# The first tile of each expert stage is started before its routing tables exist

## The chip, the cores and the metric

The kernel runs on 1 core of one Trainium2 chip. The metric is the device time of one execution in microseconds (us), as the median of several runs. Engines: PE is TensorE, DVE is VectorE, ACT is ScalarE, POOL is GpSimd, SP is the sync engine, which here only issues DMAs.

## The reference, cut to what matters

Three stages follow one another: a linear attention over 4 x 768 tokens, then a mixture of 8 experts, then a second mixture of 8 experts that takes the first one's output.

```python
x = attention(r, k, v, w, u)                   # 3072 tokens x 384
# first mixture: cosine logits; second mixture: plain logits, and a sigmoid gate besides
expert_idx = np.argmax(logits, axis=1)
for e in range(E):                             # E = 8
    mask = expert_idx == e
    h = np.maximum(x[mask] @ w1[e], 0.0)       # 384 -> 1024
    out[mask] = gate_w[mask, None] * (h @ w2[e])   # 1024 -> 384
```

A token goes to one expert. So each mixture needs the tokens sorted by expert, and the second one can't know the places of its tokens until the first has ended.

## The kernel before, in words

**Attention.** 24 units (6 chunks of 128 positions x 4 batch rows). After each chunk, DVE works out for its 512 tokens the expert (`norms1`, `choose1`, L815 to L837) and the place of each in a DRAM table `sorted1` (`place1`, L839 to L861). POOL then scatters the rows there with four indirect DMAs (`tokens`, `scatter`, L403 to L415). The last chunk's turn comes after the last unit.

**Tables.** From the totals per expert DVE builds a table of tiles (`tables`, L873 to L901): for each tile of 128 rows its expert, its offset in `sorted1`, and where the next expert's weights go. SP writes 128 padding rows behind the last row of each expert (`pads`, L308 to L313). ACT, DVE, PE and POOL wait on `tabs[m]` for the table of mixture m.

**Expert stage.** One tile is one round of a hardware loop. For tile g: ACT loads the 128 rows into `xin` (`load_rows`, L643), PE transposes them (`transpose_x`, L1291), ACT and DVE split the result in a high and a low part (`copy_xt` L650, `rest_xt` L1027), PE multiplies with the first weights (`first_product`, L1302 and L1307), ACT applies the relu (L654), PE transposes (`transpose_h`, L1317), ACT and DVE split again (`copy_ht` L659, `rest_ht` L1032), PE multiplies with the second weights (`second_product_hi` L1328, `second_product_lo` L1336), and DVE scales by the gate (`gated`, L1043). In round p, PE does `transpose_h(p)`, `first_product(p+1)`, the second product of p and `transpose_x(p+2)`. There are 27 tiles in either mixture. In mixture 1 (m = 0) each output tile is also routed for mixture 2: `transpose_y`, `logits_y`, `ranks_y` on PE, `choose` and `place_row` on DVE (L980 to L1013), and an indirect DMA into `sorted2` on POOL.

**Weights.** An expert's weights come in six pieces of 512 KB (`load_raw`, SP, L303), each into a buffer of its own. ACT writes the high part (`split_hi`, L554, about 1 us a piece) and DVE the low part (`split_lo`, L863, 1.2 us a piece); then SP may load the next expert's piece into that buffer. The first three pieces (`SOON`) hold the first weights, the last three (`LATE`) the second ones. `with_next_expert` splits `SOON` in the round of an expert's first tile and `LATE` one round later.

**The fallback.** If a test on `w` fails, all engines take a long branch (`If(bad > 0)`) that recomputes the attention in another way. The test's flag is ready at `fl_ready`. On these inputs the branch is not taken. On DVE it stands behind `tables(0)`.

The order on an engine is that of the program text, and the start of a stage reads, on ACT:

```python
act.dma_start(xin[:, :], (sorted1, sorted2)[m][0:P, :])   # after all rows have landed and the first pads
act.sem_inc(mo["ext"], 1)
act.wait_ge(tabs[m], 1)
act.wait_ge(pads_done[m], 16 * E - 16)
copy_xt(0)
load_rows(1)
```

Of the kernel before, what the change touches and what calls it, by code (L numbers as in the profile page):

```python
# [15 lines left out]
P = 128  # L16
# [53 lines left out]
def build(nc, rk_in, w_in, v_src, seq_in, uflat_in, upair_in, emb_in, epair_in, vT_in, tau_in, wall1_in, wg2_in, wall2_in, out):  # L70
# [4 lines left out]
    with ExitStack() as ctx:  # L75
# [54 lines left out]
        slot2 = sb("slot2", [P, 1], I32)  # L130

# [65 lines left out]
        pad0_done = [sem(f"pad0_done{m}") for m in range(2)]  # L197
# [7 lines left out]
        gp_chain, dve_chain, redo_chain = sem("gp_chain"), sem("dve_chain"), sem("redo_chain")  # L205
        fl_sum, fl_ps, fl_ready = sem("fl_sum"), sem("fl_ps"), sem("fl_ready")
# [59 lines left out]
        def _(sp):  # L266
# [35 lines left out]
            sp.wait_ge(gp_const, 1)  # L302
            def load_raw(k):  # L303
# [4 lines left out]
            def pads(m):  # L308

                sp.wait_ge(padaddr[m], 1)  # L310
                for e in range(E):
                    row = sp.value_load(padi[0:1, m, e:e + 1], min_val=e * CAP, max_val=e * CAP + N)
                    sp.dma_start((sorted1, sorted2)[m][bass.ds(row, P), :], padrow[:, :]).then_inc(pads_done[m] if e else pad0_done[m], 16)  # L313
# [6 lines left out]

            sp.wait_ge(fl_ready, 1)
            bad = sp.value_load(flag[0:1, 0:1], min_val=0, max_val=1)
            with sp.If(bad > 0):
# [22 lines left out]
                sp.wait_ge(padaddr[0], 2)  # L346
            with sp.Else():
                sp.nop()
            sp.nop()


            pads(0)
            for k in range(RAWS, 2 * E * RAWS):
                if k == (E + 2) * RAWS:
                    pads(1)
# [5 lines left out]
        def _(gp):  # L361
# [41 lines left out]
            def tokens(n, c, q):  # L403
                gp.wait_ge(rts[0]["slots"], n + 1)
                gp.wait_ge(row_copied, min(B * n + B, UNITS))
                gp.iota(rows[:, q, :, TOK], [[S, B]], base=c * C, channel_multiplier=1, allow_small_or_imprecise_dtypes=True).then_inc(toks, 1)
                gp.wait_ge(toks, n + 1)

# [38 lines left out]
            with gp.If(bad > 0):  # L447
# [3 lines left out]
                gp.wait_ge(tabs[0], 2)  # L451
# [32 lines left out]
        def _(act):  # L484
# [75 lines left out]
            def step(c, u, b, nu, nb):  # L560
# [18 lines left out]
                if u >= UNITS - RAWS:  # L579
                    split_hi(0, 0, u - UNITS + RAWS)  # L580
# [14 lines left out]

            LC = NCHUNK - 1
            copy_row(UNITS - 1, LC, B - 1)
# [7 lines left out]
            with act.If(bad > 0):  # L605
# [11 lines left out]
                act.wait_ge(tabs[0], 2)  # L617
# [21 lines left out]

            for m in range(2):  # L640
                mo = moes[m]

                def load_rows(g):  # L643
                    off = act.value_load(tab[0:1, m, bass.ds(g + TAB_OFF, 1)], min_val=0, max_val=SLOTS - P)
                    act.wait_ge(mo["ext"], g + 1)
                    act.dma_start(xin[:, :], (sorted1, sorted2)[m][bass.ds(off, P), :]).then_inc(mo["x_in"], 16)
# [14 lines left out]

                if m == 0:
# [3 lines left out]
                else:  # L666
                    act.wait_ge(moes[0]["sc"], 16 * last + 32)
                act.wait_ge(pad0_done[m], 16)
                act.dma_start(xin[:, :], (sorted1, sorted2)[m][0:P, :]).then_inc(mo["x_in"], 16)
                act.sem_inc(mo["ext"], 1)  # L670
                act.wait_ge(tabs[m], 1)
                last = act.value_load(tab[0:1, m, TAB_LAST:TAB_LAST + 1], min_val=E - 1, max_val=TILES - 2)
                act.wait_ge(pads_done[m], 16 * E - 16)
                copy_xt(0)
                load_rows(1)
                for n in range(2):
                    relu(0, n)
                copy_xt(1)
                load_rows(2)
                with act.Fori(0, last) as p:  # L680
                    copy_ht(p)
# [10 lines left out]
                    load_rows(p + 3)  # L692

                copy_ht(last)
                with_next_expert(act, m, last - 1, split_hi, LATE)
                if m == 0:
# [3 lines left out]
                    exps(last + 1)  # L700
                    copy_yt(last + 2)
                    keep_row(last + 2)
                    exps(last + 2)
                    with_next_expert(act, m, last, split_hi, LATE)
# [6 lines left out]
        def _(v):  # L711
# [13 lines left out]
            link(v.memset(St[:, :, :, :], 0.0))  # L725

# [49 lines left out]
            def step(c, u, b, nu, nb):  # L776
                par = b % 2

                def route():
                    if c > 0 and b == 2:  # L780
                        norms1(c - 1, c - 1)
                        choose1(c - 1)
                    if c > 0 and b == 3:
# [55 lines left out]
            def place1(n, c, q):  # L839
# [9 lines left out]
                v.wait_ge(rt["cnt"], n + 1)  # L849
                if n % NCHUNK == NCHUNK - 1:  # L850
# [575 lines left out]
```

## Time and profile before

| what | us |
| --- | --- |
| median of 3 runs | 814.78 |
| lowest and highest run | 814.62 and 816.25 |
| the profiled execution's own time | 813.74 |
| its span | 812.0 |
| PE busy | 732.1 (90% of the span) |
| DVE busy | 502.8 |
| ACT busy | 390.9 |

Times of instructions are counted from the start of the span. "Idle before" is the time for which an engine had nothing running before the instruction, with what released it behind the arrow; "issue" stands for nothing that the profile shows. A matmul at the granted clock of 1.00 runs at 2.4 GHz, at 0.50 at 1.2 GHz.

### The profile page before, as it was taken

What the parts mean: (1) busy time and instruction counts of PE and PEld (TensorE: products, weight loads), DVE (VectorE), ACT (ScalarE), POOL (GpSimd) and SP (SyncE); (2) the same over time, 40 slices, a digit from 0 to 9 for tenths busy, and PEclk for the clock granted to TensorE, in tenths of its full rate; (3) what the DMA queues carried; (4) which work ended last, traced back from release to release, by engine and by line L of the source; (5) the groups of instructions that cost most, each with busy time, mean ns of one, the idle gap of its engine ahead of it and who ended that gap; (6) DMA issues with size and microseconds to landing.
All of it is one profiled execution on the core that took longest, in us unless ns stands there. A gap on an engine that the chain in (4) does not pass through costs nothing.

```text
span 812.0 us, 21320 instructions
## 1 busy us (share of the span) xinstructions
PE 732.1 (90%) x5494; PEld 645.0 (79%) x5495; DVE 502.8 (62%) x1363; ACT 390.9 (48%) x760; POOL 159.9 (20%) x202
## 2 busy tenths in 40 slices
PE   3999899970899999999999998499999999999994
PEld 2787777760788889898888987379999999999993
DVE  7999998967467584746675665544635444436621
ACT  3666776680446463635464463144534444425521
POOL 5445565552000000000000000001000000010000
PEclk9999999895899999999999999789999999999997
DMA  6665788616433350423352433324605152415110
GB/s 130 161 160 142 203 250 232 168 61 211 181 128 116 117 183 31 150 75 109 117 178 87 141 116 117 100 88 136 202 29 194 47 184 79 157 39 194 39 33 27
DMA packets 50268, 103.75 MB, mean 128 GB/s; under 512 B 7921, under 2 KB 29904, under 8 KB 50224
## 3 DMA queue, kind: packets, MB, share of 16 engines
q1 hardware_dynamic: 29536, 67.18, 26.7%
q10 hardware_dynamic: 15568, 21.76, 10.0%
q0 software_dynamic: 5120, 14.26, 4.7%
q8 instruction: 23, 0.38, 0.2%
q14 instruction: 21, 0.17, 0.1%
HBM read 85.73 MB, written 19.01 MB: 129 GB/s over the span
## 4 chain that ended last, share of the span: by engine, by line
PE 70%; DVE 9%; issue 6%; ACT 5%; DMA 3%; ACTq 3%; SPq 1%; POOL 1%; DVEq 0%; POOLq 0%
PE bank L1302 18%; PE bank L1328 17%; PE bank L1336 10%; PE bank L1307 9%; PE bank L1317 5%; PE bank L1269 2%; ACT wall L558 2%; PE bank L1291 2%; DVE Q L755 2%; DVE SF L764 2%; DMA rk<-rk_in 2%; PE bank L1123 1%; PE bank L1110 1%; ACTq L503 1%; ACTq L245 1%
## 5 line engine op out<-in xcount | busy, mean ns | idle before, releaser
L1302 PE MATMUL bank<-wall,xT_hi 128*128 (+1 forms) x660 | 180.4, 409 | 3.0 <-ACT xT_hi L650 3.0
L1328 PE MATMUL bank<-wall,hT_hi 128*128 x880 | 165.6, 339 | 0.8 <-ACT hT_hi L659 0.5
L1328 PEld LDWEIGHTS bank<-wall,hT_hi 128*128 128x128 f32 x880 | 153.1, 188 | 7.9 <-issue 5.8
L868 DVE TENSOR_TENSOR wall<-raw,wall 128x1024 f32 (+1 forms) x96 | 112.0, 1221 | 61.9 <-ACT wall L558 58.6
L1302 PEld LDWEIGHTS bank<-wall,xT_hi 128*128 128x128 f32 x660 | 119.9, 192 | 23.9 <-issue 3.8
L654 ACT ACTIVATE hs<-bank 128x512 f32<-128x512 f32 x110 | 65.0, 591 | 110.9 <-PE bank L1307 103.8
L558 ACT ACTIVATE wall<-raw 128x1024 f32 (+1 forms) x96 | 95.0, 1050 | 42.0 <-issue 42.0
L1307 PE MATMUL bank<-wall,xT_lo 128*128 (+1 forms) x330 | 94.7, 395 | 0.0
L659 ACT ACTIVATE hT_hi<-bank 128x512 fp32r<-128x512 f32 x110 | 59.7, 595 | 70.7 <-PE bank L1317 70.7
L1336 PE MATMUL bank<-wall,hT_lo 128*128 x440 | 90.9, 348 | 0.0
L461 POOL DMA_INDIRECT sorted<-yrow,slot x28 | 27.3, 976 | 299.8 <-DVE yrow L1013 299.8
L1029 DVE TENSOR_TENSOR xT_lo<-bank,xT_hi 128x384 fp32r<-128x384 f32 x57 | 31.8, 558 | 86.9 <-ACT xT_hi L650 86.9
L475 POOL DMA_INDIRECT out<-ybuf,toki x28 | 27.3, 976 | 255.1 <-DVE ybuf L1054 255.1
L1336 PEld LDWEIGHTS bank<-wall,hT_lo 128*128 128x128 f32 x440 | 74.8, 189 | 0.0
L1307 PEld LDWEIGHTS bank<-wall,xT_lo 128*128 128x128 f32 x330 | 62.8, 190 | 14.4
L1035 DVE TENSOR_TENSOR hT_lo<-bank,hT_hi 128x512 fp32r<-128x512 f32 x110 | 70.9, 686 | 3.1 <-ACT hT_hi L659 1.6
L1317 PE MATMUL bank<-ident,hs 128*128 128x128 f32 x440 | 57.1, 272 | 1.0 <-ACT hs L654 1.0
L1317 PEld LDWEIGHTS bank<-ident,hs 128*128 128x128 f32 x440 | 51.2, 140 | 3.3 <-ACT hs L654 1.4
L1291 PE MATMUL bank<-ident,xin 128*128 128x128 f32 x171 | 28.8, 278 | 24.4 <-DMA xin<-sorted 24.4
L1110 PE MATMUL bank<-Rq,Kb 64*128 64x128 f32 x384 | 30.6, 304 | 19.6 <-DVE Kb L769 19.6
L1291 PEld LDWEIGHTS bank<-ident,xin 128*128 128x128 f32 x171 | 22.4, 143 | 31.8 <-DMA xin<-sorted 24.6
L1110 PEld LDWEIGHTS bank<-Rq,Kb 64*128 64x128 f32 x384 | 25.8, 204 | 23.6 <-issue 15.5
(194 smaller groups left out, 968.4 us busy)
## 6 DMA issues: line engine op xcount, KB each, us to landing
raw<-wall_in SPq DMA_DIRECT2D x96, 512.0 KB, 3.8
xin<-sorted ACTq DMA_DIRECT2D x59, 194.0 KB
rk<-rk_in SPq DMA_DIRECT2D x46, 192.0 KB
v_in<-v_src ACTq DMA_DIRECT2D x24, 192.0 KB, 4.3
vT<-vT_in ACTq DMA_DIRECT2D x48, 96.0 KB, 4.6
wb<-w_in SPq DMA_DIRECT2D x46, 96.0 KB
sorted<-padrow SPq DMA_DIRECT2D x16, 194.0 KB, 2.3
sorted<-yrow,slot POOLq DMA_INDIRECT x28, 2.7
```

The source lines that it names most:

```text
L558: act.activation(w_hi[:, slot, q * RAWC:(q + 1) * RAWC], raw[:, q], ACT.Copy).then_inc(w_his, 1)
L654: act.activation(hs[:, n * 512:n * 512 + 512], bank[n][:, :], ACT.Relu).then_inc(mo["h_sb"], 1)
L659: act.activation(hT_hi[:, 4 * n:4 * n + 4], bank[4 + n][:, :].rearrange("p (k t) -> p k t", k=4), ACT.Copy)\
L868: v.tensor_tensor(w_lo[:, slot, cols], raw[:, q], w_hi[:, slot, cols].bitcast(F32), ALU.subtract).then_inc(w_split, 1)
L1035: v.tensor_tensor(hT_lo[:, 4 * n:4 * n + 4], bank[4 + n][:, :].rearrange("p (k t) -> p k t", k=4), hT_hi[:, 4 * n:4 * n + 4].bitcast(F32), ...
L1110: last = pe.matmul(bank[hf][:, a * C:(a + 1) * C], Kb[q, k, a, :], Rq[q, k, a, :], start=True, stop=True, skip_group_check=True)
L1291: last = pe.transpose(bank[6][:, k * P:(k + 1) * P], xin[:, k * P:(k + 1) * P], ident[:, :])
L1302: pe.matmul(bank[n][:, :], xT_hi[:, k, :], w[:, bass.ds(slot, 1), cols].rearrange("p o n -> p (o n)"), start=(k == 0 and w is w_hi), stop= ...
L1307: last = pe.matmul(bank[n][:, :], xT_lo[:, k, :], w_hi[:, bass.ds(slot, 1), k * F + c0:k * F + c0 + 512].rearrange("p o n -> p (o n)"), st ...
L1317: last = pe.transpose(bank[4 + hf][:, j * P:(j + 1) * P], hs[:, n0:n0 + P], ident[:, :])
L1328: pe.matmul(bank[2][:, 0:DM], hT_hi[:, j, :], w[:, bass.ds(slot, 1), W2 + j * DM:W2 + (j + 1) * DM].rearrange("p o n -> p (o n)"), start=( ...
L1336: last = pe.matmul(bank[2][:, 0:DM], hT_lo[:, j, :], w_hi[:, bass.ds(slot, 1), W2 + j * DM:W2 + (j + 1) * DM].rearrange("p o n -> p (o n)" ...
```

## The change

What it does, in its parts:

- **First pads early.** SP writes padding into the first 128 rows of `sorted1` and `sorted2` at the start of the kernel.
- **Count of what the first tile needs.** In `place1` of chunks 1 to 4, DVE adds an instruction that counts for how many chunks the first expert had fewer than 128 tokens (`need`); in `place_row` it does the same for the tiles of mixture 1 (a new step 5). SP reads the counts (`need_ready`).
- **First tile.** SP, not ACT, loads the rows of tile 0 once the needed chunks or tiles have landed, without waiting for the tables. PE, ACT and DVE run all of tile 0, second product included, ahead of the wait on `tabs[m]`; the low part of its rows and of the `LATE` pieces of the first expert are made inside `tables`, behind its fifth instruction (`between`).
- **First round peeled.** The loop now starts at p = 1. What is left of round 0 stands ahead of it: load tile 1, split the `SOON` pieces of expert 1, `first_product(1)`, and so on.
- **Pads and raw weights by need.** SP issues the pads of experts 0 and 1, then raw pieces 6 to 8, waits for tile 1's rows, issues the other six pads, then the rest of the pieces. ACT waits for two pads ahead of `load_rows(1)` and for the other six ahead of `load_rows(2)`. For mixture 2, SP issues tile 0's load, all eight pads, waits for tile 1's rows, and goes on with the pieces.
- **Order.** `split_hi(0)` runs in units 16 to 21 and not 18 to 23. On DVE `split_lo(0)` runs in unit 23 and right behind it, ahead of the flag; the flag comes ahead of `norms1(5)`; the branch comes ahead of `tables(0)`. An extra Sqrt on ACT stands ahead of the last `copy_row`. POOL's iota no longer waits for `slots`.

```diff
@@ SP
+            sp.wait_ge(first_pad, 32)
+            for q in range(2):
+                for b in range(B):
+                    sp.wait_ge(landed[q][b], chunks[q])
+            sp.dma_start(xin[:, :], sorted1[0:P, :]).then_inc(moes[0]["x_in"], 16)
+            pads(0, range(2))
+            for k in range(RAWS, RAWS + len(SOON)):
+                sp.wait_ge(w_split, k - RAWS + 1)
+                load_raw(k)
+            sp.wait_ge(moes[0]["x_in"], 32)
+            pads(0, range(2, E))
+            for k in range(RAWS + len(SOON), 2 * E * RAWS):
+                if k == (E + 1) * RAWS + len(SOON):
+                    sp.wait_ge(need_ready[1], 1)
...
+                    sp.wait_ge(moes[0]["sc"], tiles)
+                    sp.dma_start(xin[:, :], sorted2[0:P, :]).then_inc(moes[1]["x_in"], 16)
+                    pads(1, range(E))
+                    sp.wait_ge(moes[1]["x_in"], 32)
                 sp.wait_ge(w_split, k - RAWS + 1)
                 load_raw(k)
@@ ACT
+            act.activation(en[:, 1:2], en[:, 0:1], ACT.Sqrt).then_inc(e_root, 1)
             copy_row(UNITS - 1, LC, B - 1)
...
+                act.sem_inc(mo["ext"], 1)
+                copy_xt(0)
+                for n in range(2):
+                    relu(0, n)
+                copy_ht(0)
                 if m == 0:
                     for q in range(2):
                         for b in range(B):
                             act.wait_ge(landed[q][b], 16 * NCHUNK // 2)
...
                 act.wait_ge(tabs[m], 1)
+                act.wait_ge(pad01_done[m], 32)
+                load_rows(1, ends[0:m])
...
+                act.wait_ge(mo["mm2"], 2)
+                for q in SOON:
+                    split_hi(E * m + 1, 1, q)
                 copy_xt(1)
+                act.wait_ge(pads_done[m], 16 * E - 32)
                 load_rows(2)
...
+                copy_xt(2)
+                load_rows(3)
+                copy_ht(1)
+                with act.Fori(1, last) as p:
@@ DVE, place1
+                if 0 < n < NCHUNK - 1:
...
+                    v.scalar_tensor_tensor(out=need[0:1, j:j + 1], in0=RANKS[0:1, (B - 1) * E:(B - 1) * E + 1], scalar=float(P),
+                                           in1=need[0:1, j:j + 1], op0=ALU.is_lt, op1=ALU.add).then_inc(needed, 1)
@@ DVE, tables
                 link(v.tensor_scalar(delta, tiles, -float(P), float(CAP), ALU.mult, ALU.add))
+                between()
                 link(v.tensor_tensor(EG, bcast_mid(iota_g[:, :], E - 1), bcast_inner(ends[:, 0:E - 1], TT), ALU.is_ge))
@@ DVE, behind the last unit
-            split_lo(0, 0, 0)
             LC = NCHUNK - 1
+            for q in (1, 2):
+                split_lo(0, 0, q)
             v.wait_ge(sq_done, UNITS)
...
             place1(LC, LC, LC % 2)
-            for q in (1, 2):
-                split_lo(0, 0, q)
-            counts1(link)
-            tables(0, link)
             with v.If(bad > 0):
...
             with v.Else():
-                v.nop()
+                relink = chained(v, tab_chain)
+                counts1(relink)
+                tables(0, relink, first_rows1)
@@ DVE, start of a stage
+                rest_ht(0)
+                keep_ext(m, 1)
+                for q in SOON:
+                    split_lo(E * m + 1, 1, q)
+                rest_xt(m, 1)
@@ PE
+                transpose_h(0)
+                second_product_hi(0, 0, E * RAWS * m, held=(m == 1))
+                second_product_lo(0, 0)
                 pe.wait_ge(tabs[m], 1)
                 transpose_x(1)
...
+                first_product(1, 0, slot, pieces)
+                if m == 0:
+                    transpose_y(1)
+                    logits_y(1)
+                first_product(1, 1, slot, pieces)
+                transpose_x(2)
+                if m == 0:
+                    ranks_y(1)
+                with pe.Fori(1, last) as p:
```

`first_rows1`, the `between` of mixture 1, is `keep_ext(0, 0)`, `rest_xt(0, 0)` and `split_lo(0, 0, q)` for the three `LATE` pieces; that of mixture 2 is the first two for m = 1 and a `with_next_expert` that splits nothing unless an expert has one tile alone.

## Rows read from the trace of the kernel before

**Rows 1.** Windows: busy us (instructions) of each engine, granted PE clock, DMA share, GB/s.
```profile
0.00:188.00 188.00, 155.41 (x2263) 128.04 (x2264) 166.84 (x413) 122.94 (x253) 101.17 (x141) 0.97 0.62 166
188.00:202.80 14.80, 0.00 (x0) 0.00 (x0) 10.75 (x27) 0.00 (x0) 4.06 (x5) 0.50 0.76 240
202.80:212.34 9.54, 7.81 (x25) 5.83 (x25) 2.27 (x10) 2.06 (x4) 0.00 (x0) 0.67 0.63 253
224.09:503.24 279.15, 276.55 (x1601) 246.88 (x1601) 176.64 (x621) 140.35 (x295) 24.40 (x25) 1.00 0.37 118
```

**Rows 2.** Timeline, end of the attention: start us, us, engine, line, [idle before <- releaser].
```profile
178.50 0.68 DVE L805 TENSOR_TENSOR YT<-bank,dv 128x512 f32<-128x512 f32 x1
179.10 1.22 DVE L868 TENSOR_TENSOR wall<-raw,wall 128x1024 fp32r<-128x1024 f32 x1
180.93 0.18 DVE L914 TENSOR_REDUCE flagp<-wbad 128x1 f32<-128x24 f32 x1 [0.61 <-ACT sqj L537]
182.53 0.18 DVE L819 RECIPROCAL r<-r 128x4 f32<-128x4 f32 x1 [1.03 <-ACT r L541]
184.86 0.19 DVE L837 TENSOR_TENSOR oh<-iota,r 128x32 fp32r<-128x32 f32 x1
187.84 0.17 DVE L859 CAST slot<-r 128x4 int32<-128x4 f32 x1
188.49 8.74 SPq L313 DMA_DIRECT2D sorted<-padrow  x8
```

**Rows 3.** Timeline, tables of mixture 1 and its first tiles.
```profile
190.28 0.15 DVE L871 TENSOR_TENSOR e<-sum,ecap 128x8 f32<-128x8 f32 x1
191.91 0.41 DVE L885 TENSOR_TENSOR cmpb<-iota_g,e 128x238 f32<-128x238 f32 x1
195.93 0.18 DVE L901 TENSOR_SCALAR tab<-tab 128x35 int32<-128x35 int32 x1
197.60 0.35 ACTq L669 DMA_DIRECT2D xin<-sorted  x1
199.44 3.50 DVE L868 TENSOR_TENSOR wall<-raw,wall 128x1024 fp32r<-128x1024 f32 x3 [3.33 <-issue]
202.80 0.90 PE L1291 MATMUL bank<-ident,xin 128*128 128x128 f32 x3 [16.35 <-DMA xin<-sorted]
204.44 2.90 PE L1302 MATMUL bank<-wall,xT_hi 128*128 128x512 f32 x6 [0.73 <-ACT xT_hi L650]
209.81 0.17 DVE L1041 COPY ext<-xin 128x2 f32<-128x2 f32 x1 [4.53 <-DMA xin<-sorted]
224.09 1.04 PE L1317 MATMUL bank<-ident,hs 128*128 128x128 f32 x8
```

**Rows 4.** Timeline, between the mixtures and first tiles of the second.
```profile
517.69 0.17 DVE L1089 CAST padi<-bank 128x8 int32<-128x8 f32 x1 [0.90 <-PE bank L1278]
518.60 7.99 SPq L313 DMA_DIRECT2D sorted<-padrow  x8
522.83 0.35 ACTq L669 DMA_DIRECT2D xin<-sorted  x1
524.72 0.18 DVE L901 TENSOR_SCALAR tab<-tab 128x35 int32<-128x35 int32 x1
525.67 0.90 PE L1291 MATMUL bank<-ident,xin 128*128 128x128 f32 x3 [8.02 <-DMA xin<-sorted]
528.87 2.90 PE L1302 MATMUL bank<-wall,xT_hi 128*128 128x512 f32 x6 [2.29 <-ACT xT_hi L650]
536.95 1.09 ACT L659 ACTIVATE hT_hi<-bank 128x512 fp32r<-128x512 f32 x2 [0.56 <-PE bank L1317]
539.79 2.96 ACT L558 ACTIVATE wall<-raw 128x1024 f32 x3 [1.76 <-issue]
545.88 1.03 PE L1317 MATMUL bank<-ident,hs 128*128 128x128 f32 x8
```

**Rows 5.** DMA issues, 180 to 225 us: KB each, median us to landing.
```profile
sorted<-padrow SPq DMA_DIRECT2D x8, 194.0 KB, 2.1
```

More of the change, by code:

```diff
@@ L318, in _ @@
                     load_raw(u - UNITS // 2)
+            sp.wait_ge(need_ready[0], 1)
+            chunks = [sp.value_load(needi[0:1, q:q + 1], min_val=16, max_val=16 * NCHUNK // 2) for q in range(2)]
             sp.wait_ge(fl_ready, 1)
@@ L638, in exps, with load_rows @@
                 act.activation(r1[:, 6:7], r1[:, 4:5], ACT.Exp, scale=-1.0).then_inc(rts[1]["ex"], 1)
+            ends = []
             for m in range(2):
                 mo = moes[m]
-                def load_rows(g):
+                def load_rows(g, before=()):
                     off = act.value_load(tab[0:1, m, bass.ds(g + TAB_OFF, 1)], min_val=0, max_val=SLOTS - P)
                     act.wait_ge(mo["ext"], g + 1)
+                    for end in before:
+                        act.wait_ge(moes[0]["sc"], 16 * end + 32)
                     act.dma_start(xin[:, :], (sorted1, sorted2)[m][bass.ds(off, P), :]).then_inc(mo["x_in"], 16)
@@ L665, in _ @@
                             act.wait_ge(landed[q][b], 16 * NCHUNK // 2)
[L666 to L670, printed above, removed]
-                act.wait_ge(tabs[m], 1)
[L672 to L677, printed above, removed]
+                act.wait_ge(tabs[m], 1)
+                act.wait_ge(pad01_done[m], 32)
+                load_rows(1, ends[0:m])
+                ends.append(act.value_load(tab[0:1, m, TAB_LAST:TAB_LAST + 1], min_val=E - 1, max_val=TILES - 2))
+                last = ends[m]
+                act.wait_ge(mo["mm2"], 2)
+                for q in SOON:
+                    split_hi(E * m + 1, 1, q)
                 copy_xt(1)
+                act.wait_ge(pads_done[m], 16 * E - 32)
                 load_rows(2)
-                with act.Fori(0, last) as p:
-                    copy_ht(p)
+                if m == 0:
+                    copy_yt(1)
+                    keep_row(1)
+                relu(1, 0)
+                if m == 0:
+                    exps(1)
+                relu(1, 1)
+                copy_xt(2)
+                load_rows(3)
+                copy_ht(1)
+                with act.Fori(1, last) as p:
                     with_next_expert(act, m, p - 1, split_hi, LATE)
@@ L700, in _ @@
                     exps(last + 1)
+                    with_next_expert(act, m, last, split_hi, LATE)
                     copy_yt(last + 2)
@@ L871, in counts1, with tables @@
                 link(v.tensor_tensor(n_e, sum8[:, :], ecap[:, :], ALU.subtract))
-            def tables(m, link):
+            def tables(m, link, between):
                 tiles, ends, delta = (e8[:, j, :] for j in range(1, 4))
@@ L1090, in _, with first_rows2 @@
                     link(v.tensor_tensor(n_e, bank[3][:, 48:48 + E], ecap[:, :], ALU.subtract))
-                    place_row(last + 2)
-                    tables(1, link)
-                    with_next_expert(v, m, last, split_lo, LATE)
+                    place_row(last + 2, final=True)
+                    def first_rows2():
+                        keep_ext(1, 0)
+                        rest_xt(1, 0)
+                        with_next_expert(v, 0, last, split_lo, LATE)
+                    tables(1, link, first_rows2)
         @block.tensor
```

136 lines of the change are left out of this document (87 added, 49 removed).

## The prediction

> **What bounds the kernel now.** I read the windows by stage first. PE is busy for 276.6 of the 279.2 us of the first mixture's rounds at a granted clock of 1.00 [rows 1], so within the rounds only less PE work would help, and the change takes none away. DVE is busy for 166.8 of the 188.0 us of the attention [rows 1]: there every DVE instruction added costs about its length. What is left are the two joins. In the first PE does nothing for 14.8 us and then runs at a mean clock of 0.67 [rows 1]. In the second it waits 8.02 us for `xin`, and then until 528.87 for the first product [rows 4].
>
> I take as the yardstick of each join the start of `transpose_h(1)`: behind it the two kernels do the same rounds. It is at 224.09 in the first [rows 3] and 545.88 in the second [rows 4]. The forecast is by how much each moves.
>
> **What ends the first join today.** The last places are written at 188.0 [rows 2]. POOL scatters, the rows land, and ACT issues tile 0's load at 197.60; it has landed at 202.80 [rows 3]. The tables are ready at 196.11 [rows 3], before the rows, so today they cost nothing. From 202.80 on PE is nearly all work: 7.81 of 9.54 us [rows 1].
>
> **First join, part by part.**
>
> *Attention.* Four added counts in `place1`, DVE instructions on one partition; the nearest row is L871 with 0.15 us [rows 3]. The fourth has a second one chained to it, 0.3 more. Sum 0.75 (nothing to 1.2). The last YT then ends at 179.95 and not 179.2. Two splits of 1.2 us [rows 2] follow at once: 182.3. Before, DVE took up the flag at 180.93 [rows 2]. So the flag starts 1.4 late and ends near 183.7, where `norms1` starts, at 182.53 before [rows 2]. From there to L837 it is 2.5 us as before, and the flag's last two instructions no longer stand behind it. The places come at 188.9, 0.9 late. The split moved into unit 23 and the extra Sqrt lie in time that DVE and ACT spend waiting; the two splits that were behind `place1` have left the way to the tables, where they hid nothing. I cost the earlier `split_hi` at nothing because DVE is the bound there; if it holds up the copy of AT, it costs at most two splits' 2 us.
>
> *Tile 0.* By the reference's own routing (worked out on its inputs) the first expert has 59, 111 and 183 tokens after one, two and three chunks, so chunks 0 to 2 suffice, long landed. SP can issue the load at about 185, once it has the flag. All of tile 0 then runs between 188 and 206, beside the scatter, and what stood between 202.80 and the second product of tile 0 leaves the path.
>
> *Tables.* These are late now. Behind L901 DVE stood for 3.33 us on nothing that the profile shows, with only the branch between it and L868 [rows 3]. I take that as the price of the branch, which now stands ahead of the tables: 189.0 + 3.3 = 192.3. L871 to L885 takes 1.6 us [rows 3], then `keep_ext` and `rest_xt` 0.7, three splits 3.5, and L885 to the end 4.2 [rows 3]: 202.4. That is 6.3 us later than before. Bounds of the branch: nothing and 3.3.
>
> The Trainium skill has a rule for this, in "Runtime: NRT & Kernel Launch", section "Instruction fetch mechanics": a taken branch to a place outside the fetched window costs a fetch. By it the 3.3 us travel with the branch and the tables stay late; without it they would be at 199.1.
>
> *Tile 1.* ACT takes 0.7 us from a semaphore to a load with an address read from a table (SP took that from L1089 to its first pad [rows 4]): issued at 203.1. A load took 2.84 us with quiet queues (522.83 to 525.67 [rows 4]) and 5.2 beside raw weights (197.60 to 202.80 [rows 3]). Pieces 6 to 8 will have landed, so 2.84: at 206.0. Before, it was there at 209.8 [rows 3].
>
> *Pads.* SP now waits for tile 1 with six pads in hand, and ACT waits for those pads ahead of `load_rows(2)`, with `copy_yt(1)`, `keep_row(1)` and both relus of tile 1 queued behind it; PE in turn stands at `logits_y(1)`. Eight pads took 8.74 and 7.99 us [rows 2, 4], so six take 6.5: 212.5. Landing adds 2.1 [rows 5], and 0.7 for the issue: tile 2's load goes out at 215.3. SP sends pieces 9 to 14 right behind the pads, so I take 5.2: 220.5. PE has stood for some 5 us before and its clock will be low (0.50 in the stretch without work [rows 1]): three transposes of 0.90 as at 202.80 [rows 3]. `transpose_h(1)` at 221.4: **2.7 us gained** of the 18 that tile 0 was started earlier. With 2.84 for that load it is 5.1, held to some 4 by `logits_y`, the product and the relu behind `copy_yt`; with the branch for nothing 6; with 5.2 us for tile 1's load too, 0.3.
>
> On loads, the Trainium skill ("DMA: Bandwidth & Descriptors", the section on the fixed cost) gives 2.0 us plus bytes over 436 GB/s, for 194 KB an estimate of 2.5 us. By it the load of tile 2 would take half of what I allow, and the gain be near 4; the row at 197.60 speaks against it where raw weights are under way.
>
> **Second join.** The count for SP is ready near 518.6, one instruction behind `place_row`'s step 4, which follows L1089 [rows 4]. Two register reads and the issue, 1.3: 519.9 against 522.83 [rows 4]. Landed 522.7. Today the first product starts 3.2 after the landing [rows 4], part of it waiting for the eighth pad; without that wait it is 1.7: 524.4, which is 4.5 earlier. Then 17.0 us of work follow as now (528.87 to 545.88 [rows 4]), 541.4. But tile 0 stands alone, and the order shows three waits that the overlapped round hides: relu, transpose and copy between its two products, 1.2 (the copies alone are 1.09 [rows 4]); `copy_xt(1)` behind three splits of together 2.96 [rows 4], of which 1.4 outlast the second product; and the low part of tile 1 behind DVE's splits with tile 2's load, issued at 538.6 beside pieces 57 to 59, 0.3. Sum 544.3: **1.6 us gained** (0.5 to 2.5).
>
> *Rounds.* Step 5 in `place_row` adds 0.2 us of DVE to each of 28 rounds. DVE is busy for 176.6 of 279.2 us [rows 1] and its results wait for PE, so nothing; if it were on the path, 5.6.
>
> **Sum.** 813.74 - 2.7 - 1.6 = 809.4 for an execution like the profiled one. That one was 1.04 below the median of the runs, 814.78. Forecast: 810.5.
>
> **The rivals.**
>
> *The branch or the loads are cheaper (0.17).* Its evidence is only one gap, at a time of heavy DMA traffic. First join 6, second 2: 806.8.
>
> *No change that can be told (0.10).* Tile 1's load takes 5.2, and the late `LATE` pieces, issued 6 to 16 us later than today, hold ACT in round 1. Gain under 1: 814. For it: six pads and six pieces of 512 KB leave SP in one burst. Against it: the pieces are needed only at 222.
>
> *Slower (0.08).* One mechanism, tile 1's rows in the first join. Everything from there is a chain of 15.4 us (206.0 to 221.4). From a landing at 208.7 that join gains nothing, from 211.9 on the whole is slower by 0.2%. It takes tables at 208, that is, a branch of 9 us, since fetch and pads share the DMA engines; 817.0 at a landing of 212.5. Against it: the branch was 3.3 us with raw loads under way.
>
> *The main case (0.65)* by itself: 808.5 to 812.8, from the bounds of the loads and counts.
>
> **The numbers.** A measurement here tells about 0.2%, 1.6 us, from nothing. The main case is faster by more than that for all but 0.04 of its chance, and so is the first rival: faster 0.79, within 0.12, slower 0.09. The range leaves out the far half of each rival: 806.0 to 813.6.
>
> **What would show it.** In the profile after: L1291 for tile 0 near 188 and 523; DVE's gap of 3 us right behind `place1` and `tabs[0]` at 202; PE idle from about 211 to 216 with ACT waiting on a pad; SP's last pad of the first mixture past 211; `transpose_h(1)` at 221.4 and 544.3, then rounds of the same length as before. Wrong would make it: tables at 199 or before (the branch is not the 3.3 us), tile 2's load landing by 218, or rounds that are longer because a changed order of splits and copies lets PE wait.

## The result, and the profile after

The changed kernel is slower. Its median is 818.40 us (11 runs), that of the kernel before 813.67 in the same measurement; the ratio of all runs is 1.0043, 95% interval 1.0024 to 1.0062 (the quotient of the two medians alone is 1.0058). Forecast were 810.5 us and a range of 806.0 to 813.6. The profiled execution has a span of 814.3 us against 812.0. One execution of `e4_rows2` below, 1216.8 us at a granted clock of 0.56, is left out of its median and ratio.

Where the 2.3 us of the profiles lie can be read from one mark in each round, the start of `transpose_h`. h(1) is that of tile 1 in mixture 1, h(26) that of its last tile, h'(1) and h'(2) those of mixture 2 (which has 28 tiles, h'(0) to h'(27), where mixture 1 has 27). Each column is the difference of two starts in the timeline of PE, so the columns add up to the span.

| profile | to h(1) | h(1) to h(2) | h(2) to h(26) | h(26) to h'(1) | h'(1) to h'(2) | rest | span |
| --- | --- | --- | --- | --- | --- | --- | --- |
| before | 224.1 | 10.9 | 268.2 | 42.6 | 9.6 | 256.6 | 812.0 |
| changed | 220.3 | 11.1 | 270.7 | 44.2 | 11.2 | 256.8 | 814.3 |

So the stretch to h(1) gained 3.8 us. The 24 rounds from h(2) to h(26), which were to stay as they were, gave 2.5 back. The second join gained nothing and lost 1.5, and the round behind it lost 1.7 more (by the unrounded starts).

**The first join.** Timeline of the changed kernel, which answers to [rows 2, 3]:

```profile
177.00 0.68 DVE L858 TENSOR_TENSOR YT<-bank,dv 128x512 f32<-128x512 f32 x1
182.69 0.21 SPq L369 DMA_DIRECT2D xin<-sorted  x1
185.66 0.16 DVE L923 CAST oh<-placed 128x8 fp32r<-128x8 f32 x1
188.00 0.88 PE L1377 MATMUL bank<-ident,xin 128*128 128x128 f32 x3 [3.56 <-issue]
188.59 0.17 DVE L933 TENSOR_TENSOR e<-sum,ecap 128x8 f32<-128x8 f32 x1 [2.76 <-issue]
198.20 0.18 DVE L964 TENSOR_SCALAR tab<-tab 128x35 int32<-128x35 int32 x1
199.28 0.37 ACTq L684 DMA_DIRECT2D xin<-sorted  x1
201.80 0.17 DVE L993 COPY ext<-xin 128x2 f32<-128x2 f32 x1 [0.49 <-DMA xin<-sorted]
202.50 6.20 SPq L320 DMA_DIRECT2D sorted<-padrow  x6
211.75 0.36 ACTq L684 DMA_DIRECT2D xin<-sorted  x1
212.16 0.49 ACT L661 ACTIVATE yT<-bank 128x384 f32<-128x384 f32 x1 [8.48 <-issue]
212.70 1.46 PE L1355 MATMUL bank<-rtW,yT 128*128 128x16 f32 x6 [5.47 <-ACT yT L661]
218.45 0.77 PE L1377 MATMUL bank<-ident,xin 128*128 128x128 f32 x3 [0.27 <-DMA xin<-sorted]
220.34 1.09 PE L1403 MATMUL bank<-ident,hs 128*128 128x128 f32 x8 [0.99 <-issue]
```

Tile 0 is transposed at 188.00 and not 202.80. The gap on DVE stands between the end of `place1` and the tables now: 2.76 us where it was 3.33 [rows 3]. The Trainium skill's rule ("Runtime: NRT & Kernel Launch", "Instruction fetch mechanics"), that a taken branch out of the fetched window costs a fetch, agrees with this: the stall went where the branch went. That the stall is a fetch, no run here shows. Then comes the chain of tile 1's load, six pads, ACT's wait of 8.48 us on nothing that the profile names, and PE's of 5.47 behind it. Of 14.8 us by which tile 0 starts earlier, 3.8 reach h(1). And 1.5 of these came before the join: the last `YT` starts at 177.00, before at 178.50 [rows 2]. It starts anywhere from 176.2 to 179.8 in the profiles below, so this is scatter. Counted from there, h(1) comes 43.3 us later where it was 45.6, which is 2.3 gained.

**The rounds.** Timeline of ACT, two rounds that split weights, changed kernel:

```profile
242.81 1.09 ACT L697 ACTIVATE hT_hi<-bank 128x512 fp32r<-128x512 f32 x2 [1.40 <-PE bank L1403]
246.03 2.96 ACT L592 ACTIVATE wall<-raw 128x1024 f32 x3 [2.13 <-issue]
248.90 0.47 ACT L661 ACTIVATE yT<-bank 128x384 f32<-128x384 f32 x1
254.89 1.09 ACT L697 ACTIVATE hT_hi<-bank 128x512 fp32r<-128x512 f32 x2 [1.44 <-PE bank L1403]
257.30 2.96 ACT L592 ACTIVATE wall<-raw 128x1024 f32 x3 [1.33 <-issue]
```

And the same two kinds of round in the kernel before:

```profile
246.60 1.09 ACT L659 ACTIVATE hT_hi<-bank 128x512 fp32r<-128x512 f32 x2 [1.41 <-PE bank L1317]
249.44 2.96 ACT L558 ACTIVATE wall<-raw 128x1024 f32 x3 [1.76 <-issue]
258.23 1.09 ACT L659 ACTIVATE hT_hi<-bank 128x512 fp32r<-128x512 f32 x2 [1.40 <-PE bank L1317]
260.33 2.96 ACT L558 ACTIVATE wall<-raw 128x1024 f32 x3 [1.02 <-issue]
```

From `copy_ht` to the first split ACT takes 2.13 or 1.33 us of "issue", before 1.76 or 1.02. The splits end 0.3 to 0.4 later, `copy_yt` is behind them, and PE waits for it. The granted clock is 1.00 over all these rounds in either profile, so it is not the clock. Waits of PE from 225 to 500 us, changed and then before:

```profile
PE bank L1355 <- ACT yT L661: 7.5, 11, 1.0
```
```profile
PE bank L1269 <- ACT yT L626: 2.6, 7, 0.4
```

(The numbers are us in total, times, longest.) The 24 rounds are of three kinds: the next expert's pieces are split in two rounds running, 7 times, and 10 rounds split nothing. In us, summed by kind:

| profile | 7 with the first splits | 7 with the second splits | 10 without |
| --- | --- | --- | --- |
| before | 81.7 | 76.9 | 109.7 |
| changed | 84.2 | 78.7 | 107.9 |
| e2_head (below) | 82.8 | 76.5 | 107.6 |
| e8_turn (below) | 84.9 | 78.5 | 110.2 |

So the 2.5 us are a net: the rounds with splits lost 4.3, and those without gained 1.8.

**The second join.** Timeline of the changed kernel, to be held against [rows 4]:

```profile
506.73 5.47 PE L1415 MATMUL bank<-wall,hT_hi 128*128 x16
519.55 0.14 DVE L1087 TENSOR_SCALAR needi<-need 1x1 int32<-1x1 f32 x1
520.97 0.33 SPq L383 DMA_DIRECT2D xin<-sorted  x1
523.26 0.90 PE L1377 MATMUL bank<-ident,xin 128*128 128x128 f32 x3 [4.41 <-DMA xin<-sorted]
524.83 2.90 PE L1388 MATMUL bank<-wall,xT_hi 128*128 128x512 f32 x6 [0.67 <-ACT xT_hi L688]
535.93 3.99 SPq L313 DMA_DIRECT2D raw<-wall_in  x6
538.16 0.34 ACTq L684 DMA_DIRECT2D xin<-sorted  x1
544.57 0.17 DVE L993 COPY ext<-xin 128x2 f32<-128x2 f32 x1 [4.54 <-DMA xin<-sorted]
546.29 1.68 PE L1403 MATMUL bank<-ident,hs 128*128 128x128 f32 x8 [1.15 <-issue]
547.62 2.75 PE L1388 MATMUL bank<-wall,xT_hi 128*128 x6
```

The first product starts 4.0 us earlier than before on the clock of the span. From h(26), which was itself 1.1 us early, it is 22.7 us and not 25.6, so 2.9. But SP sends six raw pieces from 535.93 on, and tile 2's load takes 6.4 us beside them (538.16 to 544.57). PE stands, and behind it matmuls take longer: 2.75 us for the six that take 1.64 in a round at full clock. The granted clock shows it, in the windows from h(26) to h'(1) and h'(1) to h'(2):

```profile
502.14:546.29 44.15, 30.54 (x135) 25.28 (x133) 20.50 (x80) 11.88 (x24) 2.93 (x3) 0.81 0.38 135
546.29:557.53 11.24, 11.24 (x54) 10.10 (x55) 6.13 (x9) 5.61 (x8) 0.98 (x1) 0.85 0.47 142
```

In the round PE is busy for all of 11.24 us at a clock of 0.85: a busy PE with more time for the same work is a slower PE. The 5.47 us at 506.73 are 16 matmuls that took 3.02 in the kernel before:

```profile
507.74 3.02 PE L1328 MATMUL bank<-wall,hT_hi 128*128 x16
```

They too ran at half clock, behind a gap of 1.50 us. What decides this is open. In the kernel before the gap is longer, 1.95 us, and the clock stays up. The repeat below has the half clock again, for less long (4.59 us), and its stretch h(26) to h'(1) is 1.7 us shorter. In the eleven profiles of other kernels these matmuls take 4.4 to 5.5 us, but for `e6_three` with 3.05.

### The profile page after: what moved, and what is told of

It reads as the page before. It is cut to its first block, busy times and chain, and to the rows that moved or that the text cites. A ratio compares the mean times of both kernels' runs of the same rounds, so it can differ in the third digit from the quotient of the medians.

```text
span 814.3 us, 21097 instructions
## 1 busy us (share of the span) xinstructions
PE 734.4 (90%) x5494; PEld 645.8 (79%) x5495; DVE 506.9 (62%) x1399; ACT 390.4 (48%) x761; POOL 160.1 (20%) x202
## 4 chain that ended last, share of the span: by engine, by line
PE 62%; DVE 13%; issue 9%; ACT 5%; ACTq 4%; DMA 4%; POOL 1%; SPq 1%; DVEq 0%; POOLq 0%
PE bank L1388 16%; PE bank L1415 14%; PE bank L1423 10%; PE bank L1393 8%; PE bank L1403 5%; ACT wall L592 3%; PE bank L1355 2%; DVE Q L806 2%; DVE SF L815 2%; PE bank L1377 2%; DMA xin<-sorted 2%; ACTq L249 2%; DMA rk<-rk_in 1%; ACT hT_hi L697 1%; DVE Kb L820 1%
## 5 line engine op out<-in xcount | busy, mean ns | idle before, releaser
L1388 PE MATMUL bank<-wall,xT_hi 128*128 (+1 forms) x660 | 183.0, 414 | 4.0 <-ACT xT_hi L688 2.3
L1415 PE MATMUL bank<-wall,hT_hi 128*128 (+1 forms) x880 | 168.0, 343 | 0.5 <-DVE ybuf L1124 0.5
L1415 PEld LDWEIGHTS bank<-wall,hT_hi 128*128 128x128 f32 x880 | 155.6, 190 | 3.6 <-issue 0.9
L1388 PEld LDWEIGHTS bank<-wall,xT_hi 128*128 128x128 f32 x660 | 121.8, 195 | 25.9 <-issue 5.2
L1423 PE MATMUL bank<-wall,hT_lo 128*128 (+1 forms) x440 | 91.0, 348 | 0.0
L1196 PE MATMUL bank<-Rq,Kb 64*128 64x128 f32 x384 | 28.8, 291 | 22.4 <-DVE Kb L820 22.4
L1196 PEld LDWEIGHTS bank<-Rq,Kb 64*128 64x128 f32 x384 | 24.1, 193 | 26.3 <-issue 14.8
L422 POOL TENSOR_TENSOR rkp<-rk 128x512 f32<-128x512 f32 x24 | 30.7, 1278 | 56.7 <-issue 48.9
L1066 DVE COPY r<-bank 128x16 f32<-128x16 f32 x28 | 4.8, 172 | 55.7 <-PE bank L1355 55.7
```

What stands on the lines that cost most here:

```text
L1196: last = pe.matmul(bank[hf][:, a * C:(a + 1) * C], Kb[q, k, a, :], Rq[q, k, a, :], start=True, stop=True, skip_group_check=True)
L1388: pe.matmul(bank[n][:, :], xT_hi[:, k, :], w[:, bass.ds(slot, 1), cols].rearrange("p o n -> p (o n)"), start=(k == 0 and w is w_hi), stop= ...
L1415: pe.matmul(bank[2][:, 0:DM], hT_hi[:, j, :], w[:, bass.ds(slot, 1), W2 + j * DM:W2 + (j + 1) * DM].rearrange("p o n -> p (o n)"), start=( ...
L1423: last = pe.matmul(bank[2][:, 0:DM], hT_lo[:, j, :], w_hi[:, bass.ds(slot, 1), W2 + j * DM:W2 + (j + 1) * DM].rearrange("p o n -> p (o n)" ...
```

## The experiments

All ratios are to the kernel before, measured on the same chip in the same job; the columns are those of the table above.

| run | median | ratio (95%) | to h(1) | h(1)-h(2) | h(2)-h(26) | h(26)-h'(1) | h'(1)-h'(2) | span |
| --- | --- | --- | --- | --- | --- | --- | --- | --- |
| r1_repeat | 819.57 | 1.0076 (1.0048 to 1.0105) | 221.7 | 12.4 | 270.5 | 42.5 | 11.1 | 815.0 |
| e2_head | 813.64 | 0.9998 (0.9976 to 1.0020) | 221.0 | 12.4 | 266.8 | 42.2 | 11.1 | 810.3 |
| e9_act | 817.25 | 1.0034 (1.0014 to 1.0053) | 221.1 | 12.4 | 269.8 | 42.4 | 11.2 | 813.8 |
| e10_dve | 818.38 | 1.0053 (1.0028 to 1.0077) | 220.3 | 13.4 | 270.5 | 42.4 | 11.2 | 815.0 |
| e8_turn | 821.56 | 1.0082 (1.0051 to 1.0113) | 224.8 | 11.1 | 273.6 | 44.3 | 9.6 | 820.0 |
| e3_pads | 808.45 | 0.9928 (0.9904 to 0.9953) | 214.7 | 11.3 | 270.9 | 42.4 | 12.5 | 808.5 |
| e4_rows2 | 813.30 | 1.0006 (0.9981 to 1.0032) | 222.9 | 13.5 | 270.5 | 39.6 | 11.2 | 814.6 |
| e5_raw57 | 812.67 | 0.9981 (0.9956 to 1.0007) | 219.9 | 11.3 | 270.9 | 41.4 | 10.2 | 810.5 |
| e7_filler | 816.07 | 1.0025 (1.0001 to 1.0049) | 221.0 | 12.4 | 270.6 | 46.2 | 9.7 | 816.7 |
| e6_three | 801.13 | 0.9822 (0.9784 to 0.9860) | 214.5 | 11.5 | 266.8 | 39.6 | 9.8 | 799.5 |

**r1_repeat: the changed kernel once more.** No edit.

> The changed kernel, unaltered. In its first profile three stretches lost time against the kernel before: the rounds of mixture 1 between transpose_h(1) and transpose_h(26) took 281.8 us and not 279.15 (+2.65), the end of mixture 1 took some 2.8 us more with the second product of the last tile at half clock (16 matmuls in 5.47 us and not 3.02), and the first rounds of mixture 2 lost about 2 with matmuls at half clock behind a wait of tile 2's rows. If the first loss is built into the order of the instructions and the second is the phase of the clock, a second profile has rounds of 281.8 within 0.3 again, while the second product of the last tile may take 3.0 or 5.5. If all of it is noise of one execution, the rounds come out near 279 too. Time: within 2 us of 818.4.

The rounds are as long again (270.5), so this loss belongs to the kernel. The stretch to h'(1) is 42.5, no longer than before, so about 1.7 of the 44.2 belongs to one execution: the 16 matmuls and the router's six ahead of them run at half clock for 1.4 us less. The slow first round of mixture 2 came again. And h(1) to h(2) takes 12.4 us at a granted clock of 0.86, where it took 11.1 at 1.00: PE's wait in the first join can cost 1.3 us once more in the round behind it. Five of the nine profiles below have this too.

**e2_head: the copies at the head of the loop.**

```diff
                 load_rows(3)
-                copy_ht(1)
                 with act.Fori(1, last) as p:
+                    copy_ht(p)
...
                     load_rows(p + 3)
-                    copy_ht(p + 1)
+
+                copy_ht(last)
```

and the same with `rest_ht` on DVE. No instruction is removed, and none passes another: only the loop's turn moves.

> The changed kernel with copy_ht(p) and rest_ht(p) at the head of the loop again, as before the change; all else stays. Theory A: the loop's turn on ACT and DVE used to lie in the wait for the transposed hidden tile (1.4 us idle ahead of copy_ht), and now lies between copy_ht and the splits or copy_yt, so that logits_y waits for copy_yt in the rounds with splits (7.5 us of such waits and not 2.6). Then the rounds of mixture 1 go back from 281.8 to 279.2 us, PE's wait for copy_yt to about 2.6, and the time falls by 2.6. Theory B, the rounds are longer because of the added step 5 in place_row: it is still there, so rounds stay at 281.8 and the time stays. Theory C, the clock alone makes the difference: no change beyond the scatter of runs.

The rounds fell by 3.7 us against the repeat, to 1.4 less than before the change, and the median by 5.9. Of the 3.7, 3.3 lie in the 14 rounds with splits. Step 5 of `place_row` is still there, so it is not what lengthened the rounds (theory B), and the granted clock of these rounds is 1.00 in both profiles (theory C). PE's waits for `copy_yt` fell to 5.5 us, not to 2.6: part of the gain has another source. ACT's issue ahead of the splits, in this run:

```profile
247.83 2.96 ACT L592 ACTIVATE wall<-raw 128x1024 f32 x3 [1.89 <-issue]
258.77 2.96 ACT L592 ACTIVATE wall<-raw 128x1024 f32 x3 [1.01 <-issue]
```

**e8_turn: the loop's turn alone, on the kernel before.**

```diff
                 load_rows(2)
-                with act.Fori(0, last) as p:
-                    copy_ht(p)
+                copy_ht(0)
+                with act.Fori(0, last) as p:
...
                     load_rows(p + 3)
-
-                copy_ht(last)
+                    copy_ht(p + 1)
```

and the same with `rest_ht` on DVE.

> The kernel before the change with one part of it: copy_ht and rest_ht at the end of the loop's body and the first ones ahead of the loop, no other edit. If the place of the loop's turn on ACT and DVE is what lengthens the rounds, they take 2.5 to 3.7 us more over mixture 1 (transpose_h(1) to (26): 282 and not 279.15), mostly in the rounds that split weights, PE waits 5 us longer for copy_yt, and the time is 3 to 5 us above the kernel before. Rival: only together with the peeled round or step 5 does it cost; then the rounds stay at 279.

This one part, on the kernel before, makes it slower by at least as much as the whole change does (1.0082 against 1.0043 and 1.0076, with intervals that overlap), with rounds of 273.6 and not 268.2. Of these 5.4 us, 4.8 lie in the rounds with splits. Its PE waits 5.7 us for `copy_yt` between 225 and 500. The rival, that it costs only with the peeled round or step 5, is out. Its second join is 1.6 us longer too, of which 1.4 are the clock: the last 16 matmuls take 4.39 us and not 3.02. What the turn spends its time on, no profile shows.

**e9_act and e10_dve: the turn of one engine at a time.** The edit of e2_head on ACT only, and on DVE only.

> The changed kernel with copy_ht(p) alone at the head of the loop again (ACT), rest_ht at its end. In the rounds with splits ACT's first split comes 1.32 us behind copy_ht and not 1.00, or 2.1 and not 1.76, and ends that much later ahead of copy_yt, for which PE waits. If ACT's turn is the one that counts, rounds 2 to 26 of mixture 1 take 267 us as with both at the head (unaltered 270.7), and the time is as there: 4 to 6 us less than the unaltered kernel. If DVE's turn is, nothing changes.

> The changed kernel with rest_ht(p) alone at the head of the loop again (DVE), copy_ht at its end. If ACT's turn is the one that counts, rounds 2 to 26 stay at 270.5 us and the time stays near the unaltered 818 to 820. If DVE's turn is, through its low parts that come behind ACT's, they fall to 267.

Neither engine is the one. ACT alone gives back 0.7 us of the rounds, DVE alone nothing, both 3.7. With ACT alone the first split comes 1.89 or 1.01 us behind `copy_ht`, as in e2_head, but DVE is later:

```profile
247.94 2.96 ACT L592 ACTIVATE wall<-raw 128x1024 f32 x3 [1.89 <-issue]
249.66 3.50 DVE L930 TENSOR_TENSOR wall<-raw,wall 128x1024 f32 x3 [2.77 <-ACT wall L592]
251.33 0.84 PE L1355 MATMUL bank<-rtW,yT 128*128 128x16 f32 x6 [0.63 <-ACT yT L661]
253.07 0.17 DVE L1066 COPY r<-bank 128x16 f32<-128x16 f32 x1
```

Here DVE starts its low parts 1.72 us behind ACT's first split; in the changed kernel it was 1.41 (246.03 to 247.44), in e2_head 1.47. The same round of e2_head, whose `transpose_h` stands 0.12 us earlier, has for the last line

```profile
252.72 0.17 DVE L1066 COPY r<-bank 128x16 f32<-128x16 f32 x1
```

Counted from the round's `transpose_h`, PE's `logits_y` starts at 7.0 us in both runs, so ACT's part is mended. But DVE, which takes up the logits (L1066) only behind its low parts, does so at 8.73 and not 8.50. ACT's work on them, its second relu behind that and the next `transpose_h` follow 0.2 later (12.00 and not 11.80; the changed kernel 12.07). So each engine's turn hides the other's. This is read from one round, and no run tests it.

**e3_pads: six pads ahead of the wait for tile 1.**

```diff
-            sp.wait_ge(moes[0]["x_in"], 32)
             pads(0, range(2, E))
+            sp.wait_ge(moes[0]["x_in"], 32)
```

> The changed kernel with SP's six later pads of mixture 1 ahead of the wait for tile 1's rows (two lines swapped). Theory A (the pads hold ACT, whose copy_yt(1) started at 212.16 after 8.5 us of nothing, and PE behind it): load_rows(2) goes out near 204.5 and not 211.75, PE's wait of 5.5 us ahead of logits_y(1) is gone, transpose_h(1) comes at 213 to 215 and not 220.3, and the time falls by 5 to 7 us. Rival: the load of tile 2 then runs beside the six raw pieces, lands at 211 or later, and PE waits there, so that only 3 to 4 us are gained. If the pads were hidden, nothing is gained.

h(1) comes at 214.7, 7.1 us before the repeat's, and 8.8 counted from the last `YT`; PE's wait ahead of `logits_y(1)` is 0.58 us. The load of tile 2 did take 6.6 us, to 212.85, as the rival says, but the timeline shows no wait of PE for it:

```profile
194.24 7.04 SPq L320 DMA_DIRECT2D sorted<-padrow  x6
206.22 0.36 ACTq L684 DMA_DIRECT2D xin<-sorted  x1
209.94 0.49 ACT L661 ACTIVATE yT<-bank 128x384 f32<-128x384 f32 x1 [3.52 <-PE bank L1348]
210.48 0.84 PE L1355 MATMUL bank<-rtW,yT 128*128 128x16 f32 x6 [0.58 <-ACT yT L661]
214.66 1.09 PE L1403 MATMUL bank<-ident,hs 128*128 128x128 f32 x8 [0.73 <-ACT hs L692]
```

Two swapped lines turn a kernel slower by 0.8% into one faster by 0.7%.

**e4_rows2: raw pieces held back until tile 2 of mixture 2 is there.**

```diff
-                    sp.wait_ge(moes[1]["x_in"], 32)
+                    sp.wait_ge(moes[1]["x_in"], 48)
```

> The changed kernel with SP waiting for the rows of tile 2 (not 1) of mixture 2 before it sends raw pieces 57 and on. Theory A: tile 2's load took 6.4 us (538.16 to 544.57) because six raw pieces were under way, PE stood for 1.5 us, twice, and its clock fell (six matmuls in 2.75 us and not 1.64 behind it). With the queue clear it takes 2.9 us, transpose_h(1) comes 21.5 - 2.3 = 19.2 us after the first product, the next round takes 9.6 and not 11.2, and the time falls by 3 to 4 us. Rival: the pieces that the second products of expert 1 need are then 5 us later, ACT waits for them in the next round, and it comes out even or slower by up to 2 us.

Each came true in part. The load of tile 2 takes 2.4 us (541.24 to 543.67), and the stretch to h'(1) is 2.9 shorter. But the nine pieces then go out in one burst, the DMA engines are full, and the round stays at 11.2 us, now at a clock of 1.00:

```profile
546.50:557.70 11.20, 10.42 (x56) 8.46 (x54) 6.66 (x10) 6.64 (x10) 0.98 (x1) 1.00 0.98 361
```

The median is 6.3 us below the repeat's, where theory A had 3 to 4 and the rival none. The span is only 0.3 shorter, since this profile lost 1.1 more in the stretch to h(1) and 1.1 more, at a clock of 0.79, behind it.

**e7_filler: matmuls that nothing reads, in the two gaps.**

```diff
+                def filler():
+                    for i in range(6):
+                        pe.matmul(bank[7][:, :], ones_r[:, :], w_hi[:, 0, 0:512], start=True, stop=True)
...
                 first_product(1, 1, slot, pieces)
+                if m == 1:
+                    filler()
                 transpose_x(2)
                 if m == 0:
                     ranks_y(1)
+                else:
+                    filler()
```

> The changed kernel with twelve matmuls of 512 columns that nothing reads, in mixture 2 alone: six ahead of transpose_x(2) and six behind it, where PE stands for 1.5 and 1.2 us. They are work added. Theory of the clock: the granted clock falls in these gaps and the round behind them runs in part at half of it (six matmuls in 2.75 us, not 1.64). With the gaps filled it stays up, the first round takes 9.6 and not 11.1, and although the fillers cost up to 1 us the time falls by 1 to 2. Rival: the round is long because it waits for rows and weights; then it stays at 11 with every matmul at full clock, and the time grows by up to 1 us.

The round behind the gaps takes 9.70 us and its clock is 1.00, so its 11.1 were the clock:

```profile
550.20:559.90 9.70, 9.70 (x54) 8.67 (x54) 5.86 (x8) 5.51 (x8) 0.98 (x1) 1.00 0.44 135
```

The gap ahead of tile 2's rows was not filled to its end: 1.77 us of it remained, and the clock stayed up all the same. In this profile the stretch ahead of the round is 3.7 us longer than the repeat's. Tile 2's load takes 8.2 us there (540.07 to 548.31) and not 6.4, and the last 16 matmuls of mixture 1 take 5.47 and not 4.59. Why the load is slower was not found. So the span shows no gain, and the ratio shows none for certain: its interval (1.0001 to 1.0049) overlaps those of the changed kernel (1.0024 to 1.0062 and 1.0048 to 1.0105). What the fillers show is the clock's price in the round, and no net gain.

**e5_raw57: three pieces back ahead of the pads.**

```diff
-                if k == (E + 1) * RAWS + len(SOON):
+                if k == (E + 2) * RAWS:
```

> The changed kernel, with raw pieces 57 to 59 sent ahead of tile 0 and the pads of mixture 2, where they stood before the change; SP's wait for tile 1's rows stays. In the run that held the pieces back until tile 2 was there, tile 2 was early and the next round was long instead: nine pieces of 512 KB kept the DMA engines busy for 0.98 of it. Theory: the place of these three pieces is what costs the second join its gain. Then tile 2's load takes about 5 us and not 6.4, the stretch from transpose_h(26) to transpose_h(1) of mixture 2 takes 41 to 42 us and not 42.5 to 44.2, the first round 9.6 to 10 and not 11.1, and the time falls by 2 to 3 us against the unaltered repeat. Rival: the gap is due to ACT's splits and the sequencer, and the first round stays at 11.1 with the time.

41.4 and 10.2 us: the second join now gains 1.2 us over the kernel before, although its last 16 matmuls take 5.47 us again, and the round behind it costs 0.6, at a clock of 1.00. Tile 2's load takes 3.6 us:

```profile
538.19 0.34 ACTq L684 DMA_DIRECT2D xin<-sorted  x1
541.83 0.17 DVE L993 COPY ext<-xin 128x2 f32<-128x2 f32 x1 [1.66 <-DMA xin<-sorted]
543.56 1.09 PE L1403 MATMUL bank<-ident,hs 128*128 128x128 f32 x8
```

The ratio falls below that of the changed kernel, 0.9981 against 1.0043 and 1.0076. The place of these pieces is most of what cost the second join: from the first product to h'(1) it is 18.6 us here, 18.3 in e4_rows2, 20.9 in the repeat and 21.5 in the first profile.

**e6_three: e2_head, e3_pads and e5_raw57 together.**

> All three edits on the changed kernel: copy_ht and rest_ht at the head of the loop, six pads ahead of the wait for tile 1, pieces 57 to 59 ahead of the pads of mixture 2. If the three costs are independent, their gains add up: against the unaltered repeat 6 for the loop's head, 11 for the pads, 2 to 3 for the pieces, so 800 to 803 us and a ratio to the kernel before near 0.985. If pads and loop head pay for the same scatter of runs (both fell by more than their profiles show, 4.7 and 6.5), only the profiles' sum is there: about 804 to 806.

801.13 us, ratio 0.9822 with an interval of 0.9784 to 0.9860: faster than both kernels, by 12.6 us than the one before. The three edits' ratios add up to 2.2% against the changed kernel's 1.0043, as measured; against the repeat's 1.0076 they add up to 3.2%, where 2.5% were measured. In the profile the gains over the kernel before stand in separate columns: 9.6 us to h(1), 1.4 in the rounds, 3.0 in the second join. Of these 3.0 us, 1.5 over the repeat are the clock, since the last 16 matmuls take 3.05 us here. Its second join runs through:

```profile
511.15 0.90 PE L1377 MATMUL bank<-ident,xin 128*128 128x128 f32 x3 [4.51 <-DMA xin<-sorted]
525.66 1.62 PE L1388 MATMUL bank<-wall,xT_hi 128*128 x6 [0.97 <-ACT xT_hi L688]
530.48 0.55 PE L1377 MATMUL bank<-ident,xin 128*128 128x128 f32 x3
532.35 1.09 PE L1403 MATMUL bank<-ident,hs 128*128 128x128 f32 x8 [1.32 <-issue]
```

## Why the prediction was wrong

**The step that failed is the yardstick.** It said that behind `transpose_h(1)` "the two kernels do the same rounds", and so put every stretch behind that mark at nothing. By the profiles these stretches lost about 4.5 us in the first one (0.2, 2.5, 1.7 and 0.2) and 5.5 in the repeat (1.5, 2.2, 1.5 and 0.2), out of a miss of 6.6 and 7.3 (4.3 us of gain were forecast, 2.3 and 3.0 were lost). Two things are in them.

The first is the loop's turn. The kernels do the same instructions in the same order, but the loop turns at another place. Before, the turn on ACT and DVE lay ahead of `copy_ht` and `rest_ht`, in a wait of 1.4 us for PE. Now it lies between `copy_ht` and the splits, where nothing covers it. Taken back out of the changed kernel it gives 3.7 us over 24 rounds (e2_head), and put into the kernel before, with nothing else changed, it costs 5.4 (e8_turn). The net of 2.5 is less because the rounds without splits got shorter. The second is the clock: the gaps of PE in the joins go on costing behind h(1) and h'(1), 1.3 and 1.4 us in the first round (12.4 for 11.1, 11.1 for 9.7 in e7_filler). The prediction counted a low clock for three transposes only. In its part on what each edit costs, the peeled round had no line at all. Its last paragraph named longer rounds as what would make it wrong, but gave them no chance.

**First join: right in mechanism, its size in part luck.** Forecast 2.7, measured 3.8 and 2.4; counted from the last `YT` the forecast was 3.4 and the measurement 2.3 and 2.0. The chain was the forecast one: branch, late tables, tile 1, six pads, ACT, `logits_y(1)`. Its terms were shifted, and the errors cancel. The attention ended 1.5 us earlier in this profile and not 0.75 later (after 22 units it was 0.35 late, the gain came in the last two). The branch took 2.76, and the tables were ready at 198.4 and not 202.4. The prediction had called tables at 199 a sign of a cheap branch; here they were early because the places were, at 185.8 for 188.9. Tile 1 was there at 201.8, 4.2 before the forecast, after a load of 2.5. But from there to h(1) it took 18.5 us (repeat 19.0) and not 15.4: tile 2's load took 6.7 us (211.75 to 218.43; repeat 7.4) and not 5.2, SP's first pad came 0.7 after the rows, and the last step took 1.9 and not 0.9. For a quiet load the Trainium skill's figure ("DMA: Bandwidth & Descriptors", "Anatomy of one DMA — SWDGE (gpsimd) path") gives an estimate of 2.5, and the trace agrees, though the page fits it to DMAs that GpSimd issues and ACT issues these. Beside raw weights it falls short by 4 to 5. That the pads cost most of what tile 0 gained is shown by e3_pads, 7.1 us in the profile.

**Second join: wrong.** Forecast 1.6 gained, measured 0.2 gained (repeat) or 1.5 lost. The load was issued as said, 1.28 us behind its count. That the first product started at 524.83 for 524.4 is luck: from h(26) it gained 2.9 (repeat 4.1) for a forecast 4.5, since the last tile's 16 matmuls took 2.45 (repeat 1.57) longer at half clock, and h(26) itself came 1.1 early in this profile. From the first product to h'(1) the forecast was 19.9 us, 17.0 as before and 2.9 of new waits. Measured were 21.5 and 20.9. The term that was mis-sized is the last one, 0.3 us for tile 2's load "beside pieces 57 to 59": six pieces were under way, not three, because pieces 60 to 62 go out as soon as tile 1's splits free their buffers. Without any beside the load it is 18.3 (e4_rows2), so the term was 2.7 to 3.2, and the two other waits together 1.3 and not 2.6. With three beside it, as the prediction had assumed, it is 18.6 (e5_raw57): 0.3 us was the right price for three, and the count was wrong.

**Slips that change nothing.** Tile 0 was started 14.8 us earlier by the forecast's own rows, and not 18. Mixture 1 has 27 rounds and not 28. The chances for "faster" add up to 0.78 and not 0.79.

**Sum.** By the profiles: 3.8 - 0.2 - 2.5 - 1.5 - 1.7 - 0.2 = -2.3, that is, 2.3 us lost. The rival on the slower side had another mechanism, a late tile 1; it did not happen.

**What stays open.** The medians differ by more than the profiles: 4.7 and 6.3 us for spans that differ by 2.3 and 3.0. Of the 4.7, 1.2 is that the profiled run of the changed kernel lay below its median (817.24 for 818.40), and 1.2 lies outside the spans (817.24 for 814.3, before 813.74 for 812.0). Runs of the changed kernel scatter over 813.4 to 821.9 us, and both e2_head and e3_pads lowered the median by more (5.9 and 11.1) than the span (4.6 and 6.5). What happens in the executions that were not profiled was not seen. Nor is it explained why rounds without splits take 10.8 us in the changed kernel and 11.0 before, and when the clock falls ahead of the second join: the kernel before has one profile only.

## What to carry to other kernels

A hardware loop's turn has a price, here 5.4 us in 24 rounds on two engines: put it where each engine waits anyway, and when a round is peeled or a body rotated, look at every engine's turn, since one that is hidden behind another shows nothing when it is moved alone. When work is run ahead of a wait, ask which queue now holds the next tile's transfer: here a few DMA issues that moved behind a wait (pads, raw weights) took back most of what 15 us of earlier work had won. Compare two profiles from more than one early mark: here the end of the attention moves by up to 3.5 us between profiles, and hides or feigns a gain in all that is counted from the start. Columns of one mark per round, that add up to the span, find such losses faster than the list of waits.

## What the runs showed of the hardware

- Moving the loop's turn alone, on two engines, changed 24 rounds by 5.4 us (268.2 to 273.6), with each instruction and its order the same; 4.8 of it in the 14 rounds that split weights.
- A load of 194 KB took 2.3 to 2.8 us with quiet queues, 3.6 and 5.0 beside three raw pieces of 512 KB from another engine's queue (e5_raw57, e6_three), and 6.4 to 8.2 beside six or more.
- Behind two gaps of 1.2 and 1.3 us (r1_repeat) the granted clock of the next round was 0.86 and the round took 11.1 us. With twelve unread matmuls in them it was 1.00 and 9.7, though 1.77 us of a gap remained. A gap of 1.95 us at the end of mixture 1, in the kernel before, was followed by matmuls at full clock, one of 1.50 in the changed kernel by matmuls at half.
